# Attention and two expert blocks: keys, queries and values of both units loaded in one transfer each

## The reference

```python
scores = scale * np.matmul(q, k.transpose(0, 1, 3, 2)) + bias     # bias = -slope[head] * distance
a = softmax(np.where(keep, scores, -1e9))                         # keep: 8 global keys, 96 local ones
x = np.matmul(a, v)                                               # -> (1536, 512)
h = x @ w_in                                                      # (512, 1024)
solu = h * softmax(h)
x = layernorm(solu) * g_ln @ w_out                                # (1024, 512)
h = x @ moe2_w_in                                                 # (512, 2048)
out = (h * sigmoid(h)) @ moe2_w_out                               # (2048, 512)
```

## Time and profile before

| | |
|---|---|
| median of 3 runs | 489.7 us (489.23 to 490.84) |
| profiled execution, its own time | 491.4 us |
| its span, first to last instruction | 489.4 us |
| PE busy | 480.2 us, 98% |
| VectorE, ScalarE, GpSimd busy | 302.5, 273.2, 220.5 us |
| granted TensorE clock | 1.00 throughout |
| read from memory, written | 40.69 MB, 3.15 MB |

### The profile page before, as it was taken

The page is one execution under the profiler, slowest core; times in us unless marked ns, Lnnn a source line. Parts: engine busy times, 40 slices in busy tenths (PEclk is TensorE's granted clock), DMA queues, the critical chain, the costliest instruction groups (busy, mean ns, idle before and its releaser), DMA issues.

```text
span 489.4 us, 8015 instructions
## 1 busy us (share of the span) xinstructions
PE 480.2 (98%) x2757; PEld 412.7 (84%) x2757; DVE 302.5 (62%) x729; ACT 273.2 (56%) x607; POOL 220.5 (45%) x288
## 2 busy tenths in 40 slices
PE   8889999999999999999999999999999999999997
PEld 5557888888888888888899988988999988988995
DVE  6778755585675676666575658665565546545542
ACT  5688646576576576755854454454454454344422
POOL 6427307678678679331624431444125431444200
PEclk9999999999999999999999999999999999999999
DMA  7994103533532642402222202221016202220003
GB/s 204 252 255 119 39 3 100 159 82 80 160 100 62 160 109 54 126 0 88 87 86 88 86 5 82 86 87 50 38 64 238 86 7 80 87 86 2 0 1 129
DMA packets 20522, 44.38 MB, mean 91 GB/s; under 512 B 2624, under 2 KB 8704, under 8 KB 20480
## 3 DMA queue, kind: packets, MB, share of 16 engines
q1 hardware_dynamic: 20160, 43.47, 30.4%
q10 hardware_dynamic: 320, 0.37, 0.2%
HBM read 40.69 MB, written 3.15 MB: 90 GB/s over the span
## 4 chain that ended last, share of the span: by engine, by line
PE 94%; SPq 3%; DMA 2%; issue 0%; DVE 0%; ACT 0%
PE hidden_ps L1193 24%; PE x_ps L1028 14%; PE hidden_ps L979 11%; PE score_ps L1216 9%; PE x_t_ps L1216 5%; PE x_ps L1216 5%; PE probs_t_ps L1216 5%; PE turn_ps L1216 5%; PE x_t_ps L966 4%; PE probs_t_ps L930 4%; PE turn_ps L1009 2%; DMA staged_q_raw<-q_t 2%; PE hidden_ps L996 2%; PE score_ps L898 1%; PE score_ps L899 1%; PE score_ps L919 1%
## 5 line engine op out<-in xcount | busy, mean ns | idle before, releaser
L874 POOL TENSOR_TENSOR wo_lo<-w_raw,wo_hi 128x512 fp32r<-128x512 f32 x32 | 41.4, 1316 | 145.5 <-ACT wo_hi L1463 145.5
L1475 ACT ACTIVATE act_hi<-mix_c 128x384 fp32r<-128x384 f32 x64 | 33.7, 526 | 96.5 <-DVE mix_c L1854 96.1
L732 POOL TENSOR_SCALAR probs<-probs,exp_inv 128x232 f32<-128x232 f32 x72 | 34.7, 499 | 49.3 <-DVE exp_inv L1625 48.1
L1296 ACT ACTIVATE probs<-logits,low_logit 128x232 f32<-128x232 f32 x96 | 45.5, 477 | 2.2 <-DVE low_logit L1612 1.9
L1854 DVE TENSOR_TENSOR mix_u<-hidden_ps,mix_p 128x384 f32<-128x384 f32 x16 | 8.9, 558 | 57.0 <-PE hidden_ps L1193 57.0
L1028 PE MATMUL x_ps<-w_out_hi,u_hi 128*128 128x512 f32 x96 | 40.6, 423 | 0.0
L1859 DVE TENSOR_TENSOR act_lo<-mix_c,act_hi 128x384 fp32r<-128x384 f32 x64 | 36.1, 567 | 6.3 <-ACT mix_c L1476 5.5
L1028 PE MATMUL x_ps<-w_out_hi,u_lo 128*128 128x512 f32 x96 | 37.9, 395 | 0.0
L1028 PE MATMUL x_ps<-w_out_lo,u_hi 128*128 128x512 f32 x96 | 37.5, 391 | 0.0
L979 PE MATMUL hidden_ps<-w_in_hi,x_hi 128*128 128x512 f32 x80 | 32.9, 411 | 0.0
L1612 DVE CUSTOM_DVE_ANT_0 logits<-score_ps,bias 128x232 f32<-128x232 f32 x88 | 30.6, 395 | 3.4 <-issue 3.4
(11 more groups left out here) (215 smaller groups left out, 1444.8 us busy)
## 6 DMA issues: line engine op xcount, KB each, us to landing
w_raw<-w SPq DMA_DIRECT2D x16, 1024.0 KB, 4.9
v_sb<-v_win SPq DMA_DIRECT2D x22, 224.0 KB
late_k_raw<-k_t SPq DMA_DIRECT2D x16, 232.0 KB, 4.2
k_raw<-k_t SPq DMA_DIRECT2D x14, 232.0 KB, 3.7
out<-out_sb SPq DMA_DIRECT2D x12, 256.0 KB, 2.1
w_in_raw<-w_in SPq DMA_DIRECT2D x4, 512.0 KB, 9.7
w_out_raw<-w_out SPq DMA_DIRECT2D x4, 512.0 KB, 14.3
late_q_raw<-q_t SPq DMA_DIRECT2D x16, 128.0 KB, 3.9
```

The costliest lines, as they stand in the source:

```text
L732: last = nc.gpsimd.tensor_scalar(probs[p][:, e, :], probs[p][:, e, :], exp_inv[:, p, e:e + 1], 0.0, ALU.mult, ALU.add)
L874: nc.gpsimd.tensor_tensor(wo_lo[j % 2][:, c, :], w2_raw[j % 2][:, c, BANK:2 * BANK], wo_hi[j % 2][:, c, :].bitcast(F32), ALU.subtract).the ...
L1296: last = nc.scalar.activation(probs[p][:, e, :], logits[b][:, e, :], ACT.Exp, scale=-1.0, bias=low_logit[:, b, e:e + 1], accum_out=exp_sum ...
L1475: nc.scalar.activation(act_hi[c][:, :], mix_c[c][:, :], ACT.Silu)
```

## The change

Keys and queries of tiles 0 to 4 come with one transfer each for both units: 128 partitions are filled from a view with the dimensions unit, row, column. Tile 0's are no longer cut in halves: keys come from SP's queue, queries from ACT's. Values of a tile come for both units at once, in rows of 512 words (2 KB) in place of 256; from tile 2 on they wait for all heads of the earlier tile. Weight blocks 0 and 1 are issued before tile 1's values. From tile 5 on the next tile's keys and queries of unit 0 are issued before the values. PE has one more warm-up matmul (8 in place of 7) and waits for the whole of tile 0's keys and queries. Names of semaphores and indices follow.

```diff
-    v_sb = [sb(f"v_sb{b}", [HALF_KEYS, 2, UH * DH], F32) for b in range(2)]
+    v_sb = sb("v_sb", [HALF_KEYS, 2, D], F32)
...
-    v_v = v_win.rearrange("t (c k) (u n) -> t u k c n", c=2, u=2)
+    v_v = v_win.rearrange("t (c k) n -> t k c n", c=2)
...
                 keys, queries = raw_of(t, 0)
-                for unit in range(2):
-                    sp.dma_start(keys[unit * DH:unit * DH + DH, :], k_v[t, unit]).then_inc(early_loaded[t], 16)
-                for unit in range(2):
-                    sp.dma_start(queries[unit * DH:unit * DH + DH, :], q_v[t, unit]).then_inc(early_loaded[t], 16)
+                sp.dma_start(keys[:, :], k_v[t]).then_inc(early_loaded[t], 16)
+                sp.dma_start(queries[:, :], q_v[t]).then_inc(early_loaded[t], 16)
...
-            def load_values(t, s):
+            def load_values(t):
                 if not there(t):
                     return
                 if t > 1:
-                    sp.wait_ge(pv_done, values_used(t - (2 if t == 2 else 1), s))
+                    sp.wait_ge(pv_done, PAIRS * (t if t > 2 else t - 1))
                 for rows in (slice(0, VALUE_ROWS), slice(VALUE_ROWS, HALF_KEYS)):
-                    sp.dma_start(values_of(t, s)[rows, :, :], v_v[t, s][rows]).then_inc(values_arrival(t, s)[0], 16)
+                    sp.dma_start(values_of(t)[rows, :, :], v_v[t][rows]).then_inc(values_arrival(t)[0], 16)
...
-            load_first(sp, 1)
+            sp.dma_start(staged_k_raw[:, :], k_v[0]).then_inc(early_loaded[0], 16)
             load_early(1)
-            load_values(0, 0)
-            load_values(0, 1)
+            load_values(0)
             load_weight(0)
-            load_values(1, 0)
             load_weight(1)
-            load_values(1, 1)
+            load_values(1)
             load_weight(2)
...
             for t in range(WHOLE, TILES):
-                load_values(t, 0)
                 load_keys_queries(t + 1, 0)
-                load_values(t, 1)
+                load_values(t)
                 load_keys_queries(t + 1, 1)
                 load_wide_x(t)
...
-                if t == 0 and half == 0:
-                    pe.wait_ge(first_half_loaded, 64)
-                elif t == 0 or half == 0:
-                    pe.wait_ge(early_loaded[t], 64)
+                if half == 0:
+                    pe.wait_ge(early_loaded[t], 32)
...
             pe.wait_ge(zeros_made, 1)
-            keep_warm(7)
+            keep_warm(8)
...
-            load_first(act, 0)
+            act.dma_start(staged_q_raw[:, :], q_v[0]).then_inc(early_loaded[0], 16)
```

More of the change, by code:

```diff
@@ L188, in attention_then_two_blocks @@
     next_k_raw = sb("next_k_raw", [P, UH * KEYS], F32)
-    next_v = [sb(f"next_v{s}", [HALF_KEYS, 2, UH * DH], F32) for s in range(2)]
+    next_v = sb("next_v", [HALF_KEYS, 2, D], F32)
     assert here[0] <= x1_end
@@ L270, in attention_then_two_blocks @@
     early_loaded = [sem(f"early_loaded{t}") for t in range(WHOLE)]
-    next_v_loaded = [sem("next_v_loaded0"), sem("next_v_loaded1")]
+    next_v_loaded = sem("next_v_loaded")
     early_probs_done = sem("early_probs_done")
@@ L274, in attention_then_two_blocks @@
     zeros_made = sem("zeros_made")
-    first_half_loaded = sem("first_half_loaded")
     dist_made = sem("dist_made")
     first_table_made = sem("first_table_made")
-    v_loaded = [sem("v_loaded0"), sem("v_loaded1")]
+    v_loaded = sem("v_loaded")
     w_loaded = [sem(f"w_loaded{r}") for r in range(IN_PIECES + OUT_PIECES)]
@@ L417, in score_bank, with values_of, values_arrival @@
         return early_score_ps[PAIRS * t + p] if t < 2 else score_ps[p % 2]
[L419 to L425, removed]
+    def values_of(t):
+        return next_v if t == 1 else v_sb
     def arrival(t):
         return 32 * (t - WHOLE + 1)
-    def values_arrival(t, s):
-        return (next_v_loaded[s], 32) if t == 1 else (v_loaded[s], 32 if t == 0 else 32 * t)
+    def values_arrival(t):
+        return (next_v_loaded, 32) if t == 1 else (v_loaded, 32 if t == 0 else 32 * t)
     def there(t):
@@ L544, in w_low @@
         return w_lo_done, sum(0 if m in POOL_LOWS else 1 if m < IN_PIECES else 2 for m in range(n + 1))
[L546 to L554, removed]
     with nc.Block() as block:
@@ L639, in _ @@
             load_early(3)
-            load_values(2, 0)
-            load_values(2, 1)
+            load_values(2)
             load_weight(6)
@@ L647, in _ @@
             load_wide_x(2)
-            load_values(3, 0)
-            load_values(3, 1)
+            load_values(3)
             load_wide_x(3)
             load_keys_queries(WHOLE, 1)
-            load_values(4, 0)
-            load_values(4, 1)
+            load_values(4)
             load_wide_x(4)
             for t in range(WHOLE, TILES):
-                load_values(t, 0)
                 load_keys_queries(t + 1, 0)
-                load_values(t, 1)
+                load_values(t)
                 load_keys_queries(t + 1, 1)
@@ L936, in values @@
                 s, b = unit_and_half(t, p)
-                if b == 0:
-                    pe.wait_ge(*values_arrival(t, s))
                 if p == 0:
+                    pe.wait_ge(*values_arrival(t))
                     after(pe, x_lo_done, t)
@@ L966, in products @@
                         last = nc.tensor.matmul(x_t_ps[e * DH:(e + 1) * DH, at:at + P],
-                                                values_of(t, s)[:, c, h * DH:(h + 1) * DH],
+                                                values_of(t)[:, c, (UH * s + h) * DH:(UH * s + h + 1) * DH],
                                                 probs_t_of(t, p)[:, (2 * e + c) * P:(2 * e + c + 1) * P],
```

## The result

The kernel after takes 546.36 us (median of 5 runs, 545.48 to 546.41), the kernel before beside it 490.36 (489.23 to 490.94). The ratio is 1.1142, 95% interval 1.1122 to 1.1161: 56 us slower. The profiled execution took 546.19 us, its span is 544.1 us; against the profiled execution of before (491.4, span 489.4) that is 54.8 and 54.7 us.

The account below looks back on a forecast made before the run. PE bounds the kernel before; after, early key and query loads on two DMA engines delay tile 4's scores by 48.1 us. With 2 us for the clock, +50 on 491.4 gives 541.5, median 540 us; range 522 to 580.

Parts of the forecast that it names:

- What can be won or lost: PE is busy 98%; its DMA waits total 6.1 us, none starting after 35 us, so only a few microseconds can be won.
- Two engines: Merged key and query transfers of tiles 0 to 4, 2 outermost in the source, run on 2 DMA engines; 130 ACT packets.
- The rate of an engine: Each of the two engines loading early keys and queries moves 24 GB/s, with bounds of 15.1 and 24.4.
- PE's work between arrivals: PE's 17.3, 8.2 and 11.2 us between early tiles hide behind loads of 23.3, 18.1 and 19.3 us.
- the 10 and more: Sign to look for: PE waits for DMA of 10 us and more where it had 1.1.
- SP's waits and queue: SP's waits before issuing the keys of tiles 2 and 3 (some 20 and 42.6 us) hide behind the engines' backlog.
- The clock: PE's granted clock may be lower after standing still before tile 4's scores: 2 us taken, bounds nothing and 4.
- 48.1 + 2: Tile 4's scores at 94.4 us instead of 46.32, 48.1 us later, plus 2 us for the clock: +50 us.
- The other edits: 2 KB value rows, later values from tile 5, earlier weights and one more warm-up matmul: all put at nothing.
- The crowded rate throughout: Rival: two engines on early loads at 15.1 GB/s give 594 us, or at 18 GB/s 570; chance 0.17.
- Sixteen engines: Rival: the destination's 128 partitions set the number, so early loads use all 16 engines; 488.5 us, chance 0.12.
- Engines faster than any row showed: Rival: the two engines on early loads reach 33 GB/s, tile 4 at 68.9 us; 514 us, chance 0.09.

Follow-up runs that it names:

- f3: Kernel after, with keys and queries of tiles 0 to 4 loaded from a host copy whose 128 rows are one outermost dimension: 488.47 us, ratio 0.9959.
- f11: Like f3, but each row of the copy is followed by its own length in padding: 488.37 us, ratio 0.9956.
- f6: Like f3, but the copy is 16 blocks of 8 rows with a padding row behind each, so 16 outermost: 489.35 us, ratio 0.9989.
- the row of 2, 4, 8, 16: Kernel after (2 outermost) and its versions from padded copies with 4, 8 and 16 outermost: 546.36, 511.52, 500.59 and 489.35 us.
- f8: Kernel after, but SP waits for tile 1's keys and queries before issuing tile 0's values and all that follows: 546.66 us, ratio 1.1159.
- f7: Kernel after, with 24 extra matmuls on PE in its wait for tile 4's keys and queries: 543.96 us, ratio 1.1102.
- f1: Kernel after, but keys and queries of tiles 0 to 4 by unit again, two transfers each with 64 rows outermost: 489.11 us, ratio 0.9978.

## Why the prediction was right

**What can be won or lost.** That PE had 6.1 us of waits to give, all early, held: the best versions found (f3, f11) gain some 2 us of 490.

**Two engines.** Shown, by the packets of the ACT queue, by the share of 0.12 to 0.13, by f3 and f6 (same transfer, 16 engines) and by the row of 2, 4, 8, 16. The rule of the Trainium skill ("DMA: Bandwidth & Descriptors", Why a DMA increments its semaphore by 16 and not by 1; the prediction names another heading of that page), that a copy runs on the largest number up to 16 that divides both outermost counts, agrees with all five of them. That a source of 2 against a destination of 128 would do so was an inference from transfers with 4 on both sides, and it held.

**The rate of an engine.** 24 GB/s was taken, the engines did 24.5 to 26.5 alone (49 to 53 over 2) and 25.4 in f8. Right for tile 0 (+0.4 us). For tile 1 it was the mis-sized term: 18.4 us where 15.4 were forecast, since SP had issued values and weights and 14 engines moved them beside the two. f8 shows it by taking them away. Of the 4.4 us by which tile 4 came late, 0.4 came at tile 0, 3.1 at tile 1 and 0.9 over tiles 2 to 4, which no run splits. That the sum came so near is in part luck: 2,194,432 B from 3.0 to 98.78 us are 22.9 GB/s on the mean, because a rate taken too low for two engines alone and too high for two in a crowd made up for each other.

**PE's work between arrivals.** It was put at the old 17.3, 8.2 and 11.2 us and taken to hide. It did hide, but it was longer: PE is busy 15.78, 10.62 and 13.23 us in the stretches that begin with tiles 1, 2 and 3, where it had been 13.95, 7.76 and 11.19, at clocks of 0.80, 0.68 and 0.85. So the last three waits for loads are 6.9, 8.0 and 6.3 us, not the 10 and more that the prediction named as a sign.

**SP's waits and queue.** No bubble of SP's came into the time of the kernel after, as forecast: in no microsecond from 5 to 98 us is the share under 0.12. But the issues themselves did not go as written. Tile 2's keys, put at some 20 us, were issued at 33.40, and tile 3's, put at 42.6, at 50.51: with transfers on two engines ahead of it, SP's queue holds an issue back. Its timeline:

```profile
1.18 0.70 SPq L602 DMA_DIRECT2D staged_k_raw<-k_t  x1
...
2.50 12.90 SPq L552 DMA_DIRECT2D next_q_raw<-q_t  x1
15.44 10.30 SPq L576 DMA_DIRECT2D v_sb<-v_win  x2
```

Tile 0's keys took 0.70 us to issue, tile 1's queries 12.90, and the two transfers of values behind them 10.30. So 14 engines stood idle while loads for them waited to be issued. PE's five long waits are all for keys and queries, which the two engines had in hand the whole time; what the late issues themselves cost no run tests.

**The clock.** 2 us forecast, 2.24 measured, and f7 gives 2.27 back. The mechanism was right; that the size fits so well is luck, since 2 was only the middle between nothing and 4. So the sum of 48.1 + 2 came out as 52.46 + 2.24, and the miss of the median, 546.36 against 540, is the arrivals' 4.4, the clock's 0.2 and 1.7 that were taken off because the profiled execution of before lay above its median; the one of after lies 0.2 below its own, and rounding up to 540 took 0.2 back.

**The other edits.** Put at nothing. f1, which is the change without its loss, is 1.4 us faster than before: values in rows of 2 KB, fewer transfers, the order and tile 0 in one piece together were worth a little more than nothing. The later issue of values from tile 5 on was hidden: the stretch after tile 4's scores is 443.0 us in f1 as before.

**Rivals.** The crowded rate throughout (594, or 570) did not come about; crowding struck tile 1 above all. Sixteen engines, had they been at work, were put at 488.5; f3 gave 488.47 and f1 489.11, inside that rival's own span of 487.4 to 490.5, and the near hit of f3 is luck, since its tile 0 was ready at 5.34 us and not at 6.0. Engines faster than any row showed (33 GB/s, 514 us) there were not: the two did at most 26.5 GB/s, where the best row had 24.4.

## What to carry to other kernels

Look at the outermost dimension of both sides of every transfer before merging two into one: merging two halves of 64 rows into 128 partitions turned 16 engines into 2, because the source kept a 2 in front. Count it from the profile: where each row is one packet, as here, the packets of a queue less its data rows, over its transfers, are the number of engines. If the merge is wanted, lay the data out so that the rows are one dimension. And a sum of bytes up to the last load bounds the time only while the loads are late all along; when they are late by little, each consumer's own order and each issue's wait has to be walked through, and the work between two waits priced at the clock that it will get.

## What the runs showed of the hardware

- Same 16 engines, same data, share 0.97 to 1.06, but 378 GB/s with 128 rows outermost (f3), 333 with the same and gaps (f11), 264 with 16 blocks of 8 (f6) and 233 with two transfers of 64 rows (f1), from 4 to 6 us, each read from one execution. How rows are dealt to engines seems to matter, not only over how many; which property of the dealing it is stays open, since no run changed that alone.
- With transfers on 2 engines ahead of it, an issue on SP's queue took up to 12.90 us, and a transfer meant for 16 engines waits there too; in the kernel before one issue took 0.35 to 0.6 us at the start.
- The granted clock did not fall at the same point in each execution: in PE's first wait, from 5.5 to 18.8 us, it had fallen to 0.50 by 9 us in the kernel after, and in f7, which is the same up to there, it stood at 1.00 until 24 us.
- Two engines, 25 GB/s each alone, fell to 20 on the mean of tile 1 (368,640 B in 18.4 us), of which the other 14 were busy for the last 11.
